# A retention layer and two dense layers on one core: another start-up, another order of the first dense run, and another order where the gated second layers begin

## Time and profile before

| | us |
|---|---|
| median of 3 runs | 1077.95 (1077.84 to 1080.76) |
| the profiled execution | 1079.18 |
| its span, first to last instruction | 1077.4 |
| TensorE busy | 1067.4 (99%) |
| VectorE busy | 887.7 (82%) |
| ScalarE busy | 602.3 (56%) |
| GpSimd busy | 333.8 (31%) |

### The profile page before, as it was taken

One profiled execution on the slowest core, in us unless ns is written; L12 is line 12 of the kernel. 1 busy time (PEld: TensorE's weight loads), 2 busy tenths in 40 slices (PEclk: granted clock), 3 DMA queues, 4 the chain that ended last, 5 costly groups with the idle time before them and its releaser, 6 DMA issues.

```text
span 1077.4 us, 15742 instructions
## 1 busy us (share of the span) xinstructions
PE 1067.4 (99%) x5988; PEld 894.8 (83%) x5988; DVE 887.7 (82%) x946; ACT 602.3 (56%) x902; POOL 333.8 (31%) x240
## 2 busy tenths in 40 slices
PE   8999999999999999999999999999999999999998
PEld 7888788888888888888888888788888788888898
DVE  3695999878979879889889998987886986978684
ACT  4787465466554566554674545556454555544453
POOL 0764542003540005530025554005544102544000
PEclk9999999999999999999999999999999999999999
DMA  9999648863456654455652235541225751130455
GB/s 355 361 407 412 237 157 287 243 231 118 145 187 214 207 185 138 176 217 194 215 173 103 99 137 206 204 137 66 73 61 151 256 195 61 45 112 20 140 186 183
DMA packets 80970, 196.46 MB, mean 182 GB/s; under 512 B 24448, under 2 KB 34688, under 8 KB 76032
## 3 DMA queue, kind: packets, MB, share of 16 engines
q1 hardware_dynamic: 78448, 191.24, 51.4%
q10 hardware_dynamic: 2448, 4.22, 1.0%
HBM read 152.87 MB, written 42.48 MB: 181 GB/s over the span
## 4 chain that ended last, share of the span: by engine, by line
PE 92%; DMA 3%; ACT 2%; DVE 1%; issue 1%; POOL 1%; ACTq 0%; SPq 0%; DVEq 0%; POOLq 0%
PE Y L809 13%; PE Y L810 13%; PE Y L811 13%; PE X L809 8%; PE Z L809 8%; PE X L810 8%; PE Z L810 8%; PE Z L811 8%; PE X L811 8%; DMA item_scratch<-ops 2%; PE Z L758 1%; PE Z L768 1%; ACT k_dec L925 1%; PE R L785 1%; DMA kv_sb<-qkv 1%
## 5 line engine op out<-in xcount | busy, mean ns | idle before, releaser
L670 POOL TENSOR_TENSOR w_ops<-raw_w,w_ops 128x512 fp32r<-128x512 f32 x90 | 127.1, 1412 | 494.5 <-ACT w_ops L937 494.4
L997 ACT CAST ops<-hid 128x1024 fp32r<-128x1024 f32 x147 | 154.7, 1053 | 160.8 <-PE Z L811 53.9
L1346 DVE TENSOR_TENSOR ops<-hid,ops 128x1024 fp32r<-128x1024 f32 x147 | 179.4, 1220 | 46.3 <-ACT ops L997 46.0
L670 POOL TENSOR_TENSOR w_ops<-sums_w,w_ops 128x512 fp32r<-128x512 f32 x120 | 172.6, 1441 | 129.8 <-ACT w_ops L937 129.3
L809 PE MATMUL Y<-ops,w_ops 128*128 128x512 f32 x360 | 140.4, 390 | 1.7 <-DVE hid L1542 1.6
L811 PE MATMUL Y<-ops,w_ops 128*128 128x512 f32 x360 | 140.1, 389 | 0.0
L810 PE MATMUL Y<-ops,w_ops 128*128 128x512 f32 x360 | 140.1, 389 | 0.0
L1036 ACT ACTIVATE gt<-gt 128x512 f32<-128x512 f32 x72 | 45.1, 633 | 118.3 <-DVE gt L1609 41.0
L809 PE MATMUL Y<-ops 128*128 128x512 f32 (+1 forms) x288 | 104.4, 362 | 0.0
L810 PE MATMUL Y<-ops 128*128 128x512 f32 (+1 forms) x288 | 104.4, 362 | 0.0
L811 PE MATMUL Y<-ops 128*128 128x512 f32 (+1 forms) x288 | 104.4, 362 | 0.0
(11 more groups left out here) (164 smaller groups left out, 2342.7 us busy)
## 6 DMA issues: line engine op xcount, KB each, us to landing
ops<-item_scratch SPq DMA_DIRECT2D x147, 512.0 KB, 3.8
raw_w<-w_f SPq DMA_DIRECT2D x30, 1024.0 KB, 5.0
item_scratch<-hid SPq DMA_DIRECT2D x30, 512.0 KB, 3.1
qk_sb<-qkv SPq DMA_DIRECT2D x24, 512.0 KB, 7.9
kv_sb<-qkv SPq DMA_DIRECT2D x20, 512.0 KB, 8.2
y_scratch<-hid SPq DMA_DIRECT2D x12, 512.0 KB, 5.3
raw<-y_scratch SPq DMA_DIRECT2D x3, 2048.0 KB, 9.5
raw<-w_b SPq DMA_DIRECT2D x5, 1024.0 KB, 5.0
```

What stands on the lines that cost most here:

```text
L670: nc.gpsimd.tensor_tensor(w_ops[:, k, 1], front_w_source(m, k), f32(w_ops[:, k, 0]), ALU.subtract).then_inc(w_lo, 1)
L997: nc.scalar.copy(hop_at(n)[:, 0], hid[:, 2 * g:2 * g + 2, OPERAND[k], :]).then_inc(hop_hi, 1)
L1346: nc.vector.tensor_tensor(hop[:, 1], hid[:, 2 * g:2 * g + 2, OPERAND[k], :], f32(hop[:, 0]), ALU.subtract).then_inc(hop_lo, 1)
```

## The change

- **Tables.** In place of four tables there are two inputs: `tables` (128 x 200 values, 102 KB: key decays, state decays, a triangle of ones and zeros) and `decay_rows` (32 x 896 values, 115 KB). The mask and the query decay are made on the chip: ScalarE and VectorE copy the 32 rows rounded into an fp32r tile, VectorE zeroes its other 96 rows, three fp32r matmuls of 512 columns (`rows_times`) give the mask's factors in Z and the query decay in R, and VectorE multiplies the mask's two halves by the triangle.
- **Start.** `tables` is SP's first DMA, the rows are ACT's. Loads of keys and queries now stand one place ahead of loads of keys and values. GpSimd scales the keys of chunks 0 and 1, one instruction each (`scale_first`); ScalarE begins with chunk 2. ScalarE runs one tiny activation before it waits for data. TensorE's idle matmuls go from 11, 6 and 4 to 8 and 3.
- **Stores.** Items 0 and 1 are no longer stored within the loop of loads; all 14 stores follow it, in the order 4, 5, 0, 1, 6 to 11, 2, 3, 12, 13. ScalarE rounds items 12 and 13 in the last chunk's turn.
- **First run.** In run 0 ScalarE does the seed ahead of the operand k = 3, and VectorE makes the sums of w behind the operands of slots 1 and 2, no longer ahead of those of slots 0 and 1.
- **First layer.** `relu_square` at position D goes from VectorE to ScalarE, as two instructions at the end of the front run. Three units of `units_at` for the first runs go to later slots (slot 5 now has two, and `front1_run` calls it).
- **Gated back runs.** `high_hop` 2 goes into the front run's last slot, 3 and 4 ahead of `tail`; on VectorE `low_hop` 2, two combinations and `low_hop` 3 go ahead of `tail`, `low_hop` 4 and a combination right behind it.

Declarations and the host's making of the tables are left out here.

```diff
@@ -106,7 +106,7 @@
     if m < R1:
-        first, count = ((0, 0), (0, 1), (1, 3), (4, 3), (7, 1), (8, 0), (8, 0))[slot]
+        first, count = ((0, 0), (0, 1), (1, 3), (4, 2), (6, 0), (6, 2), (8, 0))[slot]
         quads, x = (2, 3), 8 * (m - 1) + first
@@ -380,6 +389,8 @@
             at = max(at, early_at(x) - (2 if ITEMS[unit_item(u)] in SUMMED else 3))
+            if 7 * quad + unit_item(u) >= EARLY_PLACES:
+                at = NCH - 1
             if at == n:
@@ -430,16 +441,14 @@
+    sp.dma_start(tables_sb[:], tables).then_inc(tables_loaded, 16)
     load_qk(0)
-    sp.dma_start(mask_sb[:], decay_mask).then_inc(mask_loaded, 16)
     load_qk(1)
     load_kv(0)
-    sp.dma_start(decay_q_sb[:], decay_q).then_inc(decay_q_loaded, 16)
-    sp.dma_start(decay_s_sb[:], decay_s).then_inc(decay_q_loaded, 16)
-    load_kv(1)
     for n in range(2, QKR):
         load_qk(n)
-        load_kv(n)
+        load_kv(n - 1)
+    load_kv(QKR - 1)
     load_kv(QKR)
@@ -461,11 +470,9 @@
             load_early_quad(1, n - 11)
-        if n in (14, 16):
-            store_item(0, (n - 14) // 2)
     sp.wait_ge(quad_lo, 7)
     load_raw_w(1)
-    for i in range(2, 14):
+    for i in (4, 5, 0, 1, 6, 7, 8, 9, 10, 11, 2, 3, 12, 13):
         store_item(*divmod(i, 7))
@@ -664,6 +671,15 @@
 def _(pool):
+    def scale_first(n):
+
+        pool.wait_ge(kv_loaded[n], 16)
+        nc.gpsimd.tensor_tensor(
+            k_dec[:, n, :].rearrange("p (h d) -> p h d", h=H),
+            kv_sb[:, n, K, :].rearrange("p (h d) -> p h d", h=H),
+            decay_k_sb[:, n, :].unsqueeze(2).to_broadcast([P, H, D]),
+            ALU.mult).then_inc(k_first, 1)
+
     def low_w(m, k):
@@ -712,6 +728,9 @@
+    pool.wait_ge(tables_loaded, 16)
+    scale_first(0)
+    scale_first(1)
     for n in range(NCH):
@@ -777,7 +796,10 @@
             return
-        pe.wait_ge(k_scaled, (CH - 1) * b + (c + 1))
+        if n < 2:
+            pe.wait_ge(k_first, n + 1)
+        else:
+            pe.wait_ge(k_scaled, (CH - 1) * b + c - 1)
         if c == 0 and b:
@@ -790,14 +812,24 @@
         for _ in range(count):
-            nc.tensor.matmul(Z[:, 1, 0:P], y_sb[:, 0, 0:P], y_sb[:, 0, 0:P], start=True, stop=True)
+            nc.tensor.matmul(R[:, 0, 0:P], y_sb[:, 2, 0:P], y_sb[:, 2, 0:P], start=True, stop=True)
+
+    def rows_times(dst, i):
+
+        return nc.tensor.matmul(dst, rows_sb[:, DM + P * i:DM + P * i + P],
+                                rows_sb[:, 0:DM], start=True, stop=True)
     pe.wait_ge(zeroed, 1)
-    zeros(11)
+    zeros(8)
+    pe.wait_ge(rows_set, 1)
+    pe.wait_ge(rows_moving, 1)
+    pe.wait_ge(rows_padded, 1)
+    rows_times(Z[:, 0, :], 0)
+    rows_times(Z[:, 1, :], 1).then_inc(mask_made, 1)
     scores(0)
-    zeros(6)
+    rows_times(decay_q_ps, 2).then_inc(decay_placed, 1)
+    zeros(3)
     scores(1)
-    zeros(4)
     attend(0)
@@ -916,8 +948,7 @@
         act.wait_ge(kv_loaded[n % KVR], 16 * (n // KVR) + 16)
-        if n > 1:
-            act.wait_ge(chunk_done, n - 1)
+        act.wait_ge(chunk_done, n - 1)
         if n == 2:
@@ -1092,8 +1123,12 @@
             high_w(m, 6)
-        prep(0)
-        seed(run)
+        if run == 0:
+            seed(run)
+            prep(0)
+        else:
+            prep(0)
+            seed(run)
         quads(0)
@@ -1129,9 +1164,18 @@
             high_hop(bk, 1)
+            if second:
+                high_hop(bk, 2)
         if second:
...
         quads(6)
+        if not second:
+            h = hid[:, 2 * i:2 * i + 2, Dd, :]
+            act.wait_ge(c22_done, run + 1)
+            nc.scalar.activation(h, h, ACT.Relu).then_inc(relu_d, 1)
+            act.wait_ge(relu_d, m + 1)
+            nc.scalar.activation(h, h, ACT.Square).then_inc(h_d, 1)
+
     def root(t):
@@ -1147,10 +1191,12 @@
         t, ng, run = bk.t, bk.ng, bk.run
+        if bk.second:
+            high_hop(bk, 3)
+            high_hop(bk, 4)
+        tail(run - 1)
         for n in range(bk.groups):
-            if n == 0:
-                tail(run - 1)
-            if n + 2 < bk.groups:
+            if (3 if bk.second else 0) <= n < bk.groups - 2:
                 high_hop(bk, n + 2)
@@ -1207,13 +1253,14 @@
-    act.dma_start(decay_k_sb[:], decay_k).then_inc(decay_k_loaded, 16)
-    act.wait_ge(decay_k_loaded, 16)
-    scale_k(0)
-    act.wait_ge(decay_q_loaded, 32)
-    nc.scalar.copy(decay_q_ps, decay_q_sb[:]).then_inc(decay_placed, 1)
+    act.dma_start(staged_rows[0:4 * H], decay_rows).then_inc(rows_loaded, 16)
+    act.wait_ge(consts_set, 1)
+    nc.scalar.activation(warm[:], eps[:], ACT.Copy)
+    act.wait_ge(rows_loaded, 16)
+    nc.scalar.copy(rows_sb[0:4 * H, DM:], staged_rows[0:4 * H, DM:]).then_inc(rows_set, 1)
+    act.wait_ge(tables_loaded, 16)
     for n in range(NCH):
-        if n + 1 < NCH:
+        if 2 <= n + 1 < NCH:
             scale_k(n + 1)
@@ -1313,9 +1360,23 @@
-    nc.vector.memset(y_sb[:, 0, 0:P], 0.0).then_inc(zeroed, 1)
+    nc.vector.memset(y_sb[:, 2, 0:P], 0.0).then_inc(zeroed, 1)
     nc.vector.memset(eps[:], EPS).then_inc(consts_set, 1)
-    dve.wait_ge(mask_loaded, 16)
+    dve.wait_ge(zeroed, 1)
+    for lo, hi in ((32, 64), (64, P)):
+        op = nc.vector.tensor_copy(rows_sb[lo:hi].rearrange("p (a b) -> p a b", b=P),
+                                   y_sb[lo:hi, 2, 0:P].unsqueeze(1).to_broadcast([hi - lo, 7, P]))
+    op.then_inc(rows_padded, 1)
+    dve.wait_ge(rows_loaded, 16)
+    nc.vector.tensor_copy(rows_sb[0:4 * H, 0:DM], staged_rows[0:4 * H, 0:DM]).then_inc(rows_moving, 1)
+    dve.wait_ge(tables_loaded, 16)
+    dve.wait_ge(mask_made, 1)
+    for i in range(2):
+        op = nc.vector.tensor_tensor(mask_sb[:, i, :].rearrange("p (a t) -> p a t", a=PAIRS),
+                                     Z[:, i, :].rearrange("p (a t) -> p a t", a=PAIRS),
+                                     causal_sb.unsqueeze(1).to_broadcast([P, PAIRS, P]), ALU.mult)
+    op.then_inc(mask_set, 1)
+    dve.wait_ge(mask_set, 1)
     mask(0)
@@ -1431,7 +1492,7 @@
-        if m + 1 < MS and slot < 2:
+        if 0 < m < MS - 1 and slot < 2:
             sum_w(m + 1, 2 * slot)
@@ -1439,6 +1500,8 @@
                 combine(front, 3)
+        if m == 0 and slot in (1, 2):
+            sum_w(1, 2 * slot - 2)
         for quad, unit in units_at(m, slot):
@@ -1540,7 +1603,6 @@
         nc.vector.tensor_tensor(hid[:, 2 * p:2 * p + 2, Dd, :], Y[:], p5[:], ALU.add).then_inc(c22_done, 1)
-        relu_square(p, Dd, c22_done, run + 1, h_d)
         if fresh:
@@ -1552,6 +1614,7 @@
         relu_square(p, Bb, z_taken, run + 1, h_b)
+        prep(m, 5, fresh, t)
         if bk:
@@ -1645,14 +1708,21 @@
         t, ng, run = bk.t, bk.ng, bk.run
+        if bk.second:
+            low_hop(bk, 2)
+            combine_hop(bk, 0)
+            combine_hop(bk, 1)
+            low_hop(bk, 3)
+        tail(run - 1)
+        if bk.second:
+            low_hop(bk, 4)
+            combine_hop(bk, 2)
         for n in range(bk.groups):
-            if n == 0:
-                tail(run - 1)
-            if n + 2 < bk.groups:
+            if (3 if bk.second else 0) <= n < bk.groups - 2:
                 low_hop(bk, n + 2)
-            if n == 0:
+            if n == 0 and not bk.second:
                 combine_hop(bk, 0)
-            if n + 1 < bk.groups:
+            if (2 if bk.second else 0) <= n < bk.groups - 1:
                 combine_hop(bk, n + 1)
```

More of the change, by code:

```diff
@@ L119, in units_at, with build @@
     return [(quads[i // 11], i % 11) for i in range(x, x + count) if 0 <= i < 11 * len(quads)]
-def build(nc, qkv, decay_mask, decay_q, decay_s, decay_k, w_f1, w_f2, w_b, rms_g, out):
+def build(nc, qkv, decay_rows, tables, w_f1, w_f2, w_b, rms_g, out):
     x_dram = nc.dram_tensor("x_scratch", (16, P, 2, 2, P), F32, kind="Internal").ap()
@@ L159, in build @@
         kv_loaded = [sem(f"kv_loaded{i}") for i in range(KVR)]
-        mask_loaded = sem("mask_loaded")
-        decay_k_loaded = sem("decay_k_loaded")
-        decay_q_loaded = sem("decay_q_loaded")
+        rows_loaded = sem("rows_loaded")
+        tables_loaded = sem("tables_loaded")
+        rows_padded = sem("rows_padded")
+        rows_set = sem("rows_set")
+        rows_moving = sem("rows_moving")
+        mask_made = sem("mask_made")
+        mask_set = sem("mask_set")
+        k_first = sem("k_first")
         k_scaled = sem("k_scaled")
@@ L204, in build @@
         turn_scaled = sem("turn_scaled")
+        relu_d = sem("relu_d")
         p5_saved = sem("p5_saved")
@@ L241, in build @@
         mask_sb = sb("mask_sb", [P, 2, DM], scope=att)
[L242 to L244 removed]
+        tables_sb = sb("tables_sb", [P, CH * (H + PAIRS) + P], scope=att)
         state = sb("state", [P, PAIRS, D], scope=att)
@@ L1737, in decay_tables, with halves, leading @@
     scale = 1.0 / np.sqrt(D)
-    t, j = np.arange(P)[None, :], np.arange(P)[:, None]
-    mask = np.where(t >= j, gamma[:, None, None] ** np.maximum(t - j, 0), 0.0) * scale
```

(28 more changed lines are left out.)

8 lines of the change are left out of this document (5 added, 3 removed).

## The result

The changed kernel took 1074.1 us (median of 5 runs, 1073.12 to 1074.67) against 1079.28 for the kernel before (5 runs, 1077.84 to 1080.76): ratio 0.9952, 95% interval 0.9937 to 0.9967. The forecast was 1072.0 from a median of 1077.95, that is -5.9 us; measured were -5.2, from a median that now lies 1.3 higher. The time itself is 2.1 above the forecast one. The profiled execution took 1074.1 with a span of 1072.3, against 1079.18 and 1077.4.

What follows compares the result with a forecast made beforehand. TensorE was busy 1067.4 of 1077.4 us, so only its waits and slow stretches could be won, with DMA at full share in the retention. Terms: -3.6 + 1.2 - 1.8 + 0 - 1.7 = -5.9, median 1077.95 to 1072.0; range 1069.3 to 1076.0.

Steps and rivals of the forecast that it cites:

- The retention: Stretch from the start to run 0: earlier first loads and keys, no clock drop; -3.6 us, ends -1.5 and -5.0.
- how much the stream lets through: Retention loads: they come about 1.9 us earlier; slack at chunk 17 lets 3.6 of the start's 4.7 us through.
- 1.56 us for the clock: Start, chunk 2 to chunk 3: without the 2.04 us pause TensorE's clock should stay up, gaining another 1.56 us.
- Run 0: First front run: seed and later sums delay k = 4 by 0.6 and product 6; +1.2 us, ends -0.3 and +2.2.
- Run 1: Second front run: the wait for L1542 ahead of k = 6 goes; -1.8 us, ends -1.8 and 0.
- The square in 12 front runs: First layer's front runs: ScalarE gets 2 x 1.0 us, VectorE loses 1.2; 0, up to +0.3 in three places.
- Gated back runs: Their start: earlier hops save 0.7 for group 3 and 0.2 for group 2, twice; -1.7 us, ends -1.8 and 0.
- The signs: Trace marks listed in advance: early scores, no clock drop before 20, run 0 3.6 us earlier, later `save_u2`, gaps gone.
- (a): Rival, retention: the stream holds or the clock falls again; with both, retention -1.6 and 1074.0 us; chance 0.18.
- (b): Rival: run 0 is not delayed and the start keeps 4.7; -8.5 in sum, 1069.4 us; chance 0.12.
- (c): Rival, last chunk's turn: ScalarE stands for stores 0 and 1, about 10 us lost; slower, 1082 us; chance 0.06.
- (d): Rival: waits in run 1 and the gated runs stay, only the start less run 0 counts; 1075.5 us; chance 0.09.

Runs made afterwards that it cites:

- e7: Changed kernel with one more unused load of 512 KB in SP's queue, behind the load of kv of chunk 4; 1075.26 us, ratio 0.9966.
- e4: Changed kernel with hops, combinations and tail at the start of the gated back runs in the order of the kernel before; 1075.59 us, ratio 0.9968.
- e3: Changed kernel with GpSimd's first low weight half of run 1 held back until VectorE has made its first sum; 1073.17 us, ratio 0.9945.
- e9: Changed kernel with the keys of chunks 0 and 1 scaled by ScalarE again, eight instructions each; 1074.38 us, ratio 0.9953.
- e2: Changed kernel with 7 more idle matmuls between the mask's matmuls and scores of chunk 0; 1073.43 us, ratio 0.9949.
- e8: Changed kernel with the diffs of e1 and e2 together: early sums and seven more idle matmuls; 1070.35 us, ratio 0.9921.
- e1: Changed kernel with VectorE's first two sums of w for run 1 ahead of all operands of run 0, one guard narrowed; 1070.21 us, ratio 0.9920.
- e6: Changed kernel with the units of quads 2 and 3 back in the slots they had before; 1074.81 us, ratio 0.9959.
- e5: Changed kernel with the square at position D back on VectorE in the 12 front runs of the first layer; 1074.84 us, ratio 0.9958.

## Why the prediction was right, point by point

**The retention, forecast -3.6.** One trace showed -2.8, the mean of the six with this start is -3.4. The size is right against this trace of before; the picture of it was half right. Forecast were scores of chunk 3 at 14.7 to 15.5 and no clock drop; measured 14.9 to 17.0, with a drop of the granted clock in one of six. kv 0 was forecast at 8.8 and landed at 9.0 to 10.5: the first loads vary by 1.5 us between executions, which a single trace of before cannot show. The step named "how much the stream lets through" had the bound at chunk 17 with 3.6 of 4.7. The runs showed that it can bind, but mostly at chunk 4 (2.46 in e7, 1.51 in e4, 0.95 in e3), and not in most traces: from chunk 3 on TensorE needs 74.3 us, and the gain is what the start gives. An unaltered start gives 14.9 in one execution and 17.0 in another by the landing of kv 0 and by TensorE's pace ahead of it; why either varies is open. The prediction also put the 2.0 us between kv 0 and kv 1 down to the small tables between them. The traces after have such gaps, 2.2 to 2.8 us, where no small table stands. GpSimd's part of it (e9) and the bridge (e2, e8) are not seen in the time.

Here is luck as well. The forecast took 1.56 us for the clock from the trace and subtracted it from 1077.95, a time that among the 34 executions only those at 1.000 have, whose mean clock shows no such loss. Without the 1.56 its sum is -4.3, or 1073.6. The measured -5.2 is larger since the median of before rose to 1079.28 with the executions that were drawn.

**Run 0, forecast +1.2, measured +2.7.** This is the term that was mis-sized most, and past its own upper end of 2.2. The mechanism was as forecast: the weight cast on ScalarE waits for a sum now made behind the operands, and `save_u2` and L1542 are queued behind (e1: all of it gone). Missing in the sum was GpSimd's half of a weight beside VectorE's combination, 2.32 in place of 1.22, straight on this path: 1.1 us at k = 4, 0.5 at k = 6 (e3). The kernel before had such an instruction at 100.08 with 1.79 us where 0.7 is normal, so the price was to be seen; I put it at the end of the range, although the order that I listed let the two meet. The Trainium skill (SBUF — State Buffer, "Who interferes with whom") tells of an exclusive lock on a port pair that these two engines share; the trace agrees, in that the combination went from 1.22 to 2.32 beside GpSimd's 1.82.

**Run 1, forecast -1.8, measured -1.8.** Right, and the reason I gave first carries it: with the units back ahead of it 1.3 of it returns (e6). The square on ScalarE, which I had counted in, adds 0.1 here (e5).

**The square in 12 front runs, forecast 0, measured -0.8 (e5: 0.7).** The missing term. The last front run of each tile goes over into the back run, where hop 3's low half was ready just as TensorE needed it; 1.2 us less on VectorE took 0.2 to 0.35 us of small waits away at three places (e5). In the trace of before the low half ends at 180.81 and the matmul that reads it starts at 180.86, without a bracket, 0.04 us late, the next one 0.11:

```profile
179.59 1.22 DVE L1346 TENSOR_TENSOR ops<-hid,ops 128x1024 fp32r<-128x1024 f32 x1
...
180.86 0.50 PE L809 MATMUL X<-ops 128*128 128x512 f32 x1
```

Such gaps are under what is shown as idle, and I had looked only where a bracket stood.

**Gated back runs, forecast -1.7, measured -2.1** (e4: 2.2). Right, with 0.2 more in each.

**Sum.** -3.4 + 2.7 - 1.8 - 0.8 - 2.1 = -5.4 by traces, with the mean start; the spans of the two traces differ by 5.1, the medians by 5.2. The forecast of -5.9 had run 0 too cheap by 1.5 and two gains (the square, the gated back runs) too low by 1.2. That these two errors nearly cancel is luck, and so is the closeness of the sum.

**The signs.** Of what the prediction listed, these came: `save_u2` later than 11.0 us behind run 0's start (12.7), no gap before k = 6 of run 1, none before group 3 of the gated back runs. Scores of chunk 2, forecast at 11, began at 11.3 to 13.3 in the six traces with this start. Run 0 began 2.8 us earlier, not 3.6, and the clock did fall before 20. Neither sign of being wrong came: no trace shows a wait before scores of chunk 17, and the seed waited for no store.

**The rivals.** (a) the stream: it exists, and costs about 1 us on the median when a load is added (e7), but the changed kernel's trace waited for it only 0.16 us behind chunk 0. (b) no delay in run 0: that is e1, once the sums are made in VectorE's pause; it is worth 3.0 us by run 0 in the traces and 3.9 between the medians. (c) ScalarE's wait for stores 0 and 1: they landed in time (the first cast stood 0.45 behind ScalarE's own copy and not for a DMA, and the seed waited 0.32 for TensorE). (d) is out by e4 and e6.

The best kernel of the study is e1: 1070.2 us, 0.9920 of the kernel before. The guard on two quads was needed for one of these two sums only.

## What to carry to other kernels

When work is moved behind something on one engine, look on the other engines for an in-order instruction that waits for it with the critical work queued behind: here a cast of 0.6 us for the next run held this run's operand. Before a move is priced, ask whether the engine has a pause where the work could stand; VectorE stood still for 7.7 us across the start of run 0, and a guard that was wider than the data needed kept the sums out of it. And compare the same instruction in two traces all along the program: gains of 0.2 us stand in no list of waits, and a start differs by 1 us between executions of the same code. Last, look whether the one execution that was profiled is a usual one: its mean granted clock stands beside that of the others, and here the trace of before showed a loss that, by this mean, two thirds of the executions do not have.
